# The heads' outputs: V's two parts summed by TensorE against stacked identities, and scaled by VectorE out of PSUM

## What is computed

```python
q_assign = np.argmax(np.einsum('bhsd,hcd->bhsc', q_n, c_n), axis=-1)
k_assign = np.argmax(np.einsum('bhsd,hcd->bhsc', k_n, c_n), axis=-1)
mask = q_assign[:, :, :, None] == k_assign[:, :, None, :]
scores = scale * np.matmul(q, k.transpose(0, 1, 3, 2))
scores = np.where(mask, scores, -1000000000.0)
scores = scores - np.max(scores, axis=-1, keepdims=True)
attn = np.exp(scores)
attn = attn / (np.sum(attn, axis=-1, keepdims=True) + 1e-09)
return np.matmul(attn, v).astype(np.float32)
```

## Time and profile before

| | |
|---|---|
| median of 3 runs | 680.38 us (678.81 to 681.3) |
| the profiled execution | 680.13 us |
| its span, first to last instruction | 678.3 us |
| mean granted TensorE clock | 0.995 of full |
| TensorE matmuls (PE) | 661.5 us busy, 98% |
| weight loads (PEld) | 635.9 us busy, 94% |
| VectorE (DVE) | 382.3 us, 56% |
| ScalarE (ACT) | 321.7 us, 47% |
| GpSimd (POOL) | 191.7 us, 28% |

### The profile page before, as it was taken

The page is one execution under the profiler, slowest core; times in us unless marked ns, Lnnn a source line. Parts: engine busy times, 40 slices in busy tenths (PEclk is TensorE's granted clock), DMA queues, the critical chain, the costliest instruction groups (busy, mean ns, idle before and its releaser), DMA issues.

```text
span 678.3 us, 11306 instructions
## 1 busy us (share of the span) xinstructions
PE 661.5 (98%) x4050; PEld 635.9 (94%) x4050; DVE 382.3 (56%) x650; ACT 321.7 (47%) x619; POOL 191.7 (28%) x140
## 2 busy tenths in 40 slices
PE   7899899999999998999999999999999999999998
PEld 6889799999999997889999999999999999999997
DVE  6889798989899895443212212312378336661142
ACT  4787778787787884344202102202478125520010
POOL 5568254554525854106200000200243000060000
PEclk8999999999999999999999999999999999999999
DMA  6584745537473611102100000100421000000022
GB/s 217 104 196 127 182 101 119 144 76 173 79 185 79 145 47 47 47 0 94 63 1 0 1 1 0 46 0 1 140 86 55 16 1 1 1 1 1 0 94 94
DMA packets 16976, 46.92 MB, mean 69 GB/s; under 512 B 3024, under 2 KB 5072, under 8 KB 16944
## 3 DMA queue, kind: packets, MB, share of 16 engines
q1 hardware_dynamic: 16944, 46.48, 25.9%
HBM read 24.15 MB, written 3.15 MB: 40 GB/s over the span
## 4 chain that ended last, share of the span: by engine, by line
PE 95%; DVE 2%; ACT 1%; DMA 1%; issue 1%; SPq 0%
PE ps L459 20%; PE ps L457 20%; PE ps L458 20%; PE ps L497 9%; PE ps L505 5%; PE ps L489 5%; PE ps L506 5%; PE ps L490 5%; PE ps L471 3%; PE ps L512 2%; DMA kb<-oh_rows 1%; PE ps L707 1%; PE ps L480 1%; PE ps L640 1%; ACT x_t L780 0%
## 5 line engine op out<-in xcount | busy, mean ns | idle before, releaser
L780 ACT ACTIVATE pt_hi<-ps 128x384 fp32r<-128x384 f32 x192 | 85.0, 489 | 42.9 <-PE ps L497 42.0
L1100 DVE TENSOR_TENSOR pt_lo<-ps,pt_hi 128x384 fp32r<-128x384 f32 x192 | 97.3, 548 | 9.6 <-ACT pt_hi L780 8.3
L1073 DVE TENSOR_REDUCE neg_max<-ps 128x1 f32<-128x768 f32 x96 | 91.1, 950 | 20.0 <-PE ps L490 19.4
L811 ACT ACTIVATE prob<-ps,neg_max 128x768 f32<-128x768 f32 x96 | 86.8, 904 | 6.3 <-DVE neg_max L1073 6.3
L894 ACT ACTIVATE g_s<-ps 128x384 fp32r<-128x384 f32 x48 | 23.6, 492 | 138.9 <-PE ps L459 138.9
L459 PE MATMUL ps<-u_s,ch_s 128*128 128x384 f32 (+1 forms) x256 | 85.5, 334 | 0.0
L457 PE MATMUL ps<-u_s,ch_s 128*128 128x384 f32 (+1 forms) x256 | 85.5, 334 | 0.0
L458 PE MATMUL ps<-u_s,ch_s 128*128 128x384 f32 (+1 forms) x256 | 85.5, 334 | 0.0
L497 PE MATMUL ps<-ident,prob 128*128 128x128 f32 x576 | 82.4, 277 | 0.5 <-DVE pt_lo L1100 0.4
L497 PEld LDWEIGHTS ps<-ident,prob 128*128 128x128 f32 x576 | 66.5, 142 | 10.0 <-issue 2.3
L489 PE MATMUL ps<-ka,qa 128*128 128x384 f32 x192 | 70.9, 369 | 5.1 <-DMA kb<-oh_rows 3.0
(11 more groups left out here) (147 smaller groups left out, 1374.0 us busy)
## 6 DMA issues: line engine op xcount, KB each, us to landing
stage<-ch_dram SPq DMA_DIRECT2D x9, 768.0 KB, 4.4
qa<-pair_s SPq DMA_DIRECT2D x30, 192.0 KB, 3.0
ka<-pair_s SPq DMA_DIRECT2D x30, 192.0 KB, 4.0
raw<-q_dram SPq DMA_DIRECT2D x8, 384.0 KB, 4.4
raw<-k_dram SPq DMA_DIRECT2D x8, 384.0 KB, 4.6
raw_v<-v_dram SPq DMA_DIRECT2D x8, 384.0 KB, 4.3
out_dram<-act_u SPq DMA_DIRECT2D x16, 192.0 KB, 1.9
qb<-pair_s SPq DMA_DIRECT2D x15, 192.0 KB, 3.4
```

The lines of the kernel that those rows point to most:

```text
L780: return act.activation(o, i, ACT.Copy)
L811: act.activation(prob[:, slot, :].rearrange("p (c k) -> p c k", c=2), ps[:, 2 * slot:2 * slot + 2, 0:HS], ACT.Exp, bias=neg_max[:, s:s + 1 ...
L1073: dve.tensor_reduce(neg_max[:, s:s + 1], ps[:, 2 * slot2:2 * slot2 + 2, 0:HS], AX.XY, ALU.max, negate=True).then_inc(s_max, 1)
L1100: dve.tensor_tensor(pt_lo[at], ps[:, 4 + u, 0:HS].rearrange("p (k q) -> p k q", k=HT), pt_hi[at], ALU.subtract).then_inc(s_pt_lo, 1)
```

## The change

- **TensorE.** A constant `fold` [128, 64], two identities one below the other, is made by GpSimd at the start as the sum of the two halves of `ident`. `o_transpose` is now three matmuls with an `o_t` block as the stationary operand and `fold` as the moving one: each transposes its block and adds the two parts of V, into 64 columns of bank 6. TensorE's first instruction waits for `fold`.
- **VectorE.** `half_out` and its `o_sum` are gone. `x_out` moves here from GpSimd: it reads the 192 sums from bank 6 and multiplies by `rden` into `x_tok`, in half_out's place.
- **Denominators.** `den` is laid out rotated by three (`DEN`), so that the second half of a head and the first half of the next lie side by side, and `denominators` is called at `t == 2`, just ahead of the `x_out` there: 17 calls in place of 16.
- **Semaphores.** `s_x` takes the place of `s_x_bank`; VectorE waits for GpSimd no more.
- **GpSimd.** Its 32 multiplies and their waits are gone.

```diff
@@ gpsimd
+            pool.wait_ge(s_const, 7)
+            pool.tensor_tensor(fold[:], ident[:, 0:D], ident[:, D:P], ALU.add).then_inc(s_fold, 1)
...
-            def x_out(p, j, half, n):
-
-                pool.wait_ge(s_x_bank, n + 1)
-                pool.wait_ge(s_rden, 2 * p + j + 1)
-                pool.tensor_tensor(x_tok[:, bass.ds(p * NT + half * HT, HT), j * D:(j + 1) * D], o_sum[:, half, :, :],
-                                   rden[:, j, half * HT:half * HT + HT].unsqueeze(2).broadcast_to([P, HT, D]),
-                                   ALU.mult).then_inc(s_x, 1)
...
                 if not first:
                     split_v(p, 1)
-                    x_out(p - 1, 1, 1, 4 * p - 1)
-                x_out(p, 0, 0, 4 * p)
                 if not last:
                     split_v(p + 1, 0)
                 for n in weights[0:1]:
                     split_weights(n)
-                x_out(p, 0, 1, 4 * p + 1)
                 if scaled:
                     scale_q(p + 2)
                 for n in weights[1:2]:
                     split_weights(n)
-                x_out(p, 1, 0, 4 * p + 2)
@@ tensor
             def o_transpose():
                 for i in range(HT):
-                    mm = pe.transpose(ps[:, 6, i * P:(i + 1) * P], o_t[:, i * P:(i + 1) * P], ident[:])
+                    mm = pe.matmul(ps[:, 6, i * D:(i + 1) * D], o_t[:, i * P:(i + 1) * P], fold[:],
+                                   start=True, stop=True)
                 mm.then_inc(s_ott, 1)
...
                 if part == 0:
-                    pe.wait_ge(s_x_bank, n - 1)
+                    pe.wait_ge(s_x, n - 1)
                 weighted_v(1 - j, 1, part)
...
+            pe.wait_ge(s_fold, 1)
             pe.wait_ge(s_same_head, 4)
@@ scalar
-                               ACT.Exp, bias=neg_max[:, s:s + 1], accum_out=den[:, s:s + 1]).then_inc(s_exp, 1)
+                               ACT.Exp, bias=neg_max[:, s:s + 1], accum_out=den[:, DEN[s]:DEN[s] + 1]).then_inc(s_exp, 1)
@@ vector
-            def half_out(n, half):
-
-                dve.wait_ge(s_ott, n + 1)
-                dve.tensor_reduce(o_sum[:, half, :, :], ps[:, 6, 0:HS].rearrange("p (t a d) -> p t d a", t=HT, a=2),
-                                  AX.X, ALU.add).then_inc(s_x_bank, 1)
-
-            def denominators(h, j):
-                dve.tensor_scalar(rden[:, j, :], den[:, NT * j:NT * j + NT], 1e-9, None, ALU.add).then_inc(s_den, 1)
-                dve.wait_ge(s_den, h + 1)
-                dve.reciprocal(rden[:, j, :], rden[:, j, :]).then_inc(s_rden, 1)
+            def denominators(s0, s1, h):
+                dve.tensor_scalar(rden[:, s0:s1], den[:, s0:s1], 1e-9, None, ALU.add).then_inc(s_den, 1)
+                dve.wait_ge(s_den, h + 1)
+                dve.reciprocal(rden[:, s0:s1], rden[:, s0:s1]).then_inc(s_rden, 1)
+
+            def x_out(p, j, half, n, h):
+                dve.wait_ge(s_ott, n + 1)
+                dve.wait_ge(s_rden, h + 1)
+                s0 = DEN[NT * j + HT * half]
+                dve.tensor_tensor(x_tok[:, bass.ds(p * NT + half * HT, HT), j * D:(j + 1) * D],
+                                  ps[:, 6, 0:HT * D].rearrange("p (t d) -> p t d", t=HT),
+                                  rden[:, s0:s0 + HT].unsqueeze(2).broadcast_to([P, HT, D]),
+                                  ALU.mult).then_inc(s_x, 1)
...
-                    if t == 0 and not (first and j == 0):
-                        denominators(2 * p + j - 1, 1 - j)
+                    if t == 2:
+                        denominators(HT if first and j == 0 else NT * j, NT * j + NT, 2 * p + j)
                     if t == 2 and not (first and j == 0):
-                        if not (first and j == 1):
-                            dve.wait_ge(s_x, n - 2)
-                        half_out(n - 1, 1)
+                        x_out(p if j else p - 1, 1 - j, 1, n - 1, 2 * p + j)
                     if t == 5:
-                        if not (first and j == 0):
-                            dve.wait_ge(s_x, n - 1)
-                        half_out(n, 0)
+                        x_out(p, j, 0, n, 2 * p + j)
```

More of the change, by code:

```diff
@@ L55, in clustered_mixer @@
         identb = sb(ctx, "identb", [P, P], BF16)
+        fold = sb(ctx, "fold", [P, D], F32)
         half_pi = sb(ctx, "half_pi", [P, 1], F32)
@@ L64, in clustered_mixer @@
             o_t = sb(a0, "o_t", [P, HS], F32)
-            o_sum = sb(a0, "o_sum", [P, 2, HT, D], F32)
         act_u = sb(ctx, "act_u", [P, NC_ * CH], F32)
@@ L86, in clustered_mixer @@
                 den = sb(a1, "den", [P, 12], F32)
-                rden = sb(a1, "rden", [P, 2, NT], F32)
+                rden = sb(a1, "rden", [P, 12], F32)
                 cen_t = sb(a1, "cen_t", [P, 2, P], F32)
@@ L173, in clustered_mixer @@
         s_x = sem("s_x")
-        s_x_bank = sem("s_x_bank")
+        s_fold = sem("s_fold")
         s_stage = [sem("s_stage0"), sem("s_stage1")]
@@ L260, in weights_lo @@
             eng.tensor_tensor(lo, stage_ap(n), hi, ALU.subtract).then_inc(w_split[n], 1)
+        DEN = [(s + HT) % 12 for s in range(12)]
         Y_BANK = ((4, 5, 6, 7), (4, 5, 6, 7), (0, 2, 1, 3), (4, 5, 6, 7))
@@ L434, in _ @@
             pair(NP - 1, scaled=False, last=True, weights=W_CH1[2:3])
-            x_out(NP - 1, 1, 1, 4 * NP - 1)
             pool.wait_ge(s_x, 4 * NP)
@@ L547, in first_half_v @@
                     if prev:
-                        pe.wait_ge(s_x_bank, n)
+                        pe.wait_ge(s_x, n)
                 weighted_v(j, 0, part)
@@ L609, in _ @@
             pe.wait_ge(s_pt_lo, 12 * 2 * NP)
-            pe.wait_ge(s_x_bank, 4 * NP - 1)
+            pe.wait_ge(s_x, 4 * NP - 1)
             weighted_v(1, 1, 0)
@@ L650, in _ @@
                     elif n == 2:
-                        pe.wait_ge(s_x_bank, 4 * NP - 1)
+                        pe.wait_ge(s_x, 4 * NP)
                     elif n == 3:
@@ L1123, in _ @@
             pair(NP - 1, last=True)
-            denominators(2 * NP - 1, 1)
+            denominators(0, HT, 2 * NP)
             def x_lo(b, t):
@@ L1141, in _ @@
                 x_lo(0, t)
-            dve.wait_ge(s_x, 4 * NP - 2)
-            half_out(4 * NP - 1, 1)
+            x_out(NP - 1, 1, 1, 4 * NP - 1, 2 * NP)
             for b in range(B):
```

## The result

| | before | changed |
|---|---|---|
| median of 4 runs, us | 679.98 (678.81 to 681.3) | 691.49 (691.21 to 691.8) |
| ratio, 95% interval | | 1.0159 (1.0134 to 1.0183) |
| profiled execution, us (span) | 680.13 (678.3) | 691.21 (689.4) |

The forecast was 683.6 us with a range that ended at 688.2. The sign was right, the size was not: +11.1 us in the profiled span, where +3.5 was forecast.

A forecast was written before the change was run, and what follows sets the result against it. TensorE, with matmuls in 98% of the span, was taken as the bound. On 680.13 us: -0.9 up to 76.85, +8.2 for halves 6 to 29, -3.9 waits, -0.2 half 30, +0.3 half 31: +3.5, 683.6; range 681.0 to 688.2.

The forecast's parts named there:

- The denominators keep their 0.18 + 0.19: VectorE: the addition of 1e-9 and the reciprocal keep their 0.18 and 0.19 us, but leave slots 0 and 6.
- the lateness of 0.2 at slots 2 and 8: VectorE's next row maximum comes 0.2 us later; costed at nothing, covered by 2.7 idle us a pair; uncovered, 3.2 in all.
- The sign for being wrong: Block under 0.6 us, pair growing under 0.4 or over 1.2, or a new wait for `rden` or behind slots 2 and 8.
- Nothing is absorbed: Rival: waits behind `o_transpose` move along with VectorE's later row maximum at slots 2 and 8; without the 3.9, 687.5 us; chance 0.16.
- The fold's block: TensorE, `o_transpose`, 32 times: six passes at 0.111 us, 0.67 in place of 0.32, +0.34 a half; x192 records.
- the rival of the moving columns: Rival at `o_transpose`: moving columns set the pace, block stays 0.32 us; 677.8 us; chance 0.07, shared with the one-record rival.
- What falls into waits: TensorE: 0.41 us of a pair's 4 x 0.34 absorbed behind `o_transpose`; 0.25 goes with the one-hot step's wait where present.
- GpSimd and pair 1: Without two early GpSimd multiplies all that follows is 0.93 us earlier; TensorE's 3.03 wait for one-hot rows ends 0.9 earlier.
- GpSimd's freedom is worth more: Rival: earlier splits and copies keep loads off the one-hot rows in pair 1; -2.5 us for -0.9, 682.0 us; chance 0.14.
- Start and mixers: TensorE's first matmul at 3.07 us is not delayed, `fold` being ready by 2.5; the mixers are not touched: no cost.
- Half 30 and 31: Attention's end: half 30's +0.34 us is absorbed and its VectorE step gives -0.2; half 31, in the token mixer, costs +0.3.
- The sum: Whole kernel: -0.9, +8.2, -3.9, -0.2 and +0.3 us, together +3.5 on the profiled 680.13, giving 683.6; chance 0.6.

The follow-up runs named there:

- e5: Changed kernel with GpSimd's wait for `rden` put back ahead of each pair's first weights, in all pairs but the first: 684.93 us, ratio 1.0058.
- e1: Changed kernel without the addition of 1e-9 to the denominators, the reciprocal reading `den` itself: 683.98 us, ratio 1.0044 to the kernel before.
- e4: e1 with three transposes against `ident` again in place of the fold, the multiply reading only the high parts' sums: 677.43 us, ratio 0.9952.
- e7: Kernel before the change without the addition of 1e-9, the reciprocal reading `den` itself: 680.72 us, ratio 1.0003.
- e9: e1 with `fold` and `o_t` as F32R, so the fold takes one pass and `o_t` is rounded: 677.59 us, ratio 0.9952.
- e11: Kernel before with TensorE's fold, `half_out` copying 192 sums, GpSimd's multiplies kept, and no addition of 1e-9: 686.65 us, ratio 1.0086.

## Why the prediction was wrong, step by step

- **The step that failed** is in the part on VectorE: "The denominators keep their 0.18 + 0.19", and with it the lateness of 0.2 at slots 2 and 8 that was costed "at nothing". The denominators take 0.88 + 0.19 in the mean, and up to 2.25 + 0.19. The cover named for the lateness was VectorE's 2.7 idle us in a pair. At slot 2 it holds (up to 1.24 us in e5), at slot 8 it does not: 0.79 there costs 0.54 a pair, and the 2.14 and 2.25 of pairs 6 and 7 cost 4.1 together. That is 7.5 us of the 11.5 measured. The 0.2 was short even without a hold: from the addition to the next row maximum e5 has 0.90 us (137.53 to 138.43), where the reduce had 0.47 (136.27 to 136.74), 0.43 later; that much costs nothing, as its pair equals e1's. The reason was in the change itself: taking `x_out` from GpSimd also takes its wait for `rden`, which the prediction counted only as idle time that goes.
- **The sign for being wrong** that the prediction named, a new wait for `rden` or behind slots 2 and 8, came: TensorE waits for the multiply of L1078 (5.1 us in four waits), ScalarE for the row maximum. No rival had the hold. "Nothing is absorbed" named the path that it took, later row maxima at slots 2 and 8, but with no more than the 0.2 as their lateness; it ends nearest, at 687.5. The changed kernel's pair, 1.42 longer, looks like its 1.36 by accident: e1's, with the same blocks, is only 0.88 longer.
- **The fold's block** was right: six loads, x192, 0.67 us, which also decides against the rival of the moving columns (0.43 or less):

```profile
129.04 0.75 PEld L503 LDWEIGHTS ps<-fold,o_t 128*128 128x128 f32 x6
129.71 0.19 PEld L480 LDWEIGHTS ps<-ka,qa 128*128 128x128 f32 x1
```

- **What falls into waits** was nearly right: forecast 4 x 0.34 - 0.41 - 0.25 = 0.70 a pair, measured 30.79 - 29.91 = 0.88 in e1, where the hold is absent. Behind `o_transpose` 0.32 is absorbed (e4) for the 0.41, and the rest of the change gives 29.91 - 29.75 = 0.16 for the 0.25; e7 gets 0.14 by the missing addition alone. With the hold it is 31.33 - 29.91 = 1.42, outside the 0.4 to 1.2 that I had set. The wait for the one-hot step in regular pairs is gone, as forecast.
- **GpSimd and pair 1** had the right start and end, and a wrong link between them. The split of pair 2 comes 0.75 earlier (55.92), and the copy of one-hot rows lands at 75.90, where the forecast had the wait end. But the prediction read it as the last of eleven issues that all move with the first. It moves with ScalarE's one-hot rows instead: it is issued 2.03 later than before (73.16 for 71.13), and takes 2.74 us for 5.60, because the loads are out of its way. That is the mechanism of the rival "GpSimd's freedom is worth more", and that the end fits the forecast is luck. In e1, without the hold, half 6 starts 1.27 earlier, 0.9 forecast. In the changed kernel half 5 is 2.03 later than before (73.84 for 71.81), of which e1 shows 0.90; so TensorE comes after the data, the wait is gone, and half 6 is only 0.38 earlier.
- **Start and mixers** cost nothing, as forecast. **Half 30 and 31** cannot be told apart from the rest, but from half 25 to the mixers e1 takes 1.0 more than before.
- **The sum** without the failed step: e1's span is 3.9 above that of before, forecast 3.5. The terms err in both directions, so part of this is luck: -1.3 up to half 6 for -0.9, +4.1 from there to half 25 where the terms give about 3.3 (19 x 0.34, less 3.2 absorbed), +1.0 behind it for 1.1.
- **The moving columns** as a rival are refuted by the block above and by e9: half the columns in one pass are no faster than a transpose. By the Trainium skill ("TensorE: Matmul & The Clock Gate", section "Back-to-back issue gap") 64 columns would issue in fewer cycles than 128; the same section says that its figures at few columns leave the weight loads out. Here each pass has its own weight load and both take 0.11 us, so for this stream the measurement decides, and the prediction was right not to go by the table.

## What to carry to other kernels

A wait that you remove was also a separation in time: list what the freed engine will now run beside the instructions that it used to wait for, and price those anew. Before you carry a duration over, take its group's least, median and longest, and if they differ list every one with what ran beside it; one 474 among fifteen of 158 ns was the whole case in small, and e5's median of 163 hides eight long ones. When two runs differ by more than their waits do, read the granted clock of the stretch behind the wait. And test an instruction that is cheap in busy time but stands ahead of a critical one by leaving it out alone.

## What the runs showed that I had not expected

- A VectorE tensor_scalar of six columns takes 0.16 us, or 0.47 to 3.34 us when it starts behind a GpSimd tensor_tensor: it ends 0.02 to 0.03 us after it. A tensor_tensor with two SBUF inputs is held as well (0.79), a reciprocal of the same columns is not (0.18), nor is a multiply with one input in PSUM (0.35).
- Three passes with a weight load each take 0.33 us with 64 moving columns (e9) and with 128: halving the columns bought nothing, halving the passes bought 6.4 us.
- TensorE's wait in pair 1 brings a granted clock of half with it in four of the eight traces of the table, which costs 1.5 to 2.8 us on top of the wait.
- In e11 the same program took about 684.4, 686.7 or 688.7 us. The profiled one, 688.76, has a stretch at half clock in pair 1. Runs with no such stretch, a shorter one and this one would fit the steps, but the other four were not profiled, so this is not shown; and why the clock fell in e7 and not in the kernel before is open.
